# Scores computed transposed, with keys on partitions, in the attention stage of an attention and two-FFN kernel on Trainium2

## The reference

```python
batch, n_heads, seq, head_dim = (4, 8, 576, 64)
q_rot, k_rot = (rotate(q), rotate(k))            # RoPE over halves of 32
scores = np.matmul(q_rot, k_rot.transpose(0, 1, 3, 2)) / np.sqrt(64)
scores = scores - np.max(scores, axis=-1, keepdims=True)
attn = np.exp(scores)
attn = attn / (np.sum(attn, axis=-1, keepdims=True) + 1e-09)
x = np.matmul(attn, v)                           # to [2304 tokens, 512]
x = (x @ w_in1 - np.tanh(x @ w_in1)) @ w_out1    # w_in1 512x2048, w_out1 2048x512
h = x @ w_in2
out = (h * (1.0 / (1.0 + np.exp(-h)))) @ w_out2
```

## Time and profile before

| | before |
|---|---|
| median of 3 runs | 1187.12 us (1184.62 to 1188.59) |
| profiled execution, first to last instruction | 1186.9 us |
| PE busy | 1118.7 us, 94% |
| PE weight loads busy | 1043.8 us, 88% |
| DVE busy | 610.9 us, 51% |
| ACT busy | 521.9 us, 44% |
| POOL busy | 263.0 us, 22% |
| moved by DMA | 50.86 MB |

### The profile page before, as it was taken

How to read it: one execution, slowest core, us unless ns; L and a number is a source line. 1 busy time by engine, 2 the same in 40 slices (tenths; PEclk the granted TensorE clock), 3 DMA queues, 4 the chain that set the end, 5 groups by cost and what they waited for, 6 DMA issues and landing times.

```text
span 1186.9 us, 18468 instructions
## 1 busy us (share of the span) xinstructions
PE 1118.7 (94%) x6560; PEld 1043.8 (88%) x6560; DVE 610.9 (51%) x969; ACT 521.9 (44%) x1128; POOL 263.0 (22%) x171
## 2 busy tenths in 40 slices
PE   2899999999988899999999999999999999999998
PEld 2778888888868899999999999989998989989897
DVE  5899999999976632322323234762323223232322
ACT  3888989898961232232323232222323222232322
POOL 4556564647145500000000003550000000000000
PEclk9999999999998899999999999989999999999999
DMA  5242423233222300000000000320000000000000
GB/s 174 64 112 68 110 67 106 76 93 89 65 86 84 111 32 1 1 0 0 0 0 0 0 0 29 113 71 1 27 0 27 0 0 27 0 27 0 27 0 27
DMA packets 44493, 50.86 MB, mean 43 GB/s; under 512 B 25376, under 2 KB 25648, under 8 KB 44464
## 3 DMA queue, kind: packets, MB, share of 16 engines
q1 hardware_dynamic: 44464, 50.49, 14.2%
HBM read 36.83 MB, written 4.79 MB: 35 GB/s over the span
## 4 chain that ended last, share of the span: by engine, by line
PE 81%; DVE 6%; DMA 4%; ACT 4%; issue 3%; SPq 1%; POOL 1%; ACTq 0%; DVEq 0%; POOLq 0%
PE ps L557 33%; PE ps L576 17%; PE ps L571 16%; PE ps L443 5%; DMA Vk<-Uk 4%; PE ps L417 3%; PE ps L467 3%; PE ps L468 2%; ACT P L694 2%; PE ps L399 1%; DVE g_l L1029 1%; PE ps L421 1%; DVE negmax L886 1%; DVE pt_l L876 1%; DVE pt_r L881 1%
## 5 line engine op out<-in xcount | busy, mean ns | idle before, releaser
L557 PE MATMUL ps<-xs_h,win_l 128*128 128x384 f32 x768 | 260.7, 339 | 2.7 <-DVE xs_l L946 2.7
L557 PE MATMUL ps<-xs_h,win_h 128*128 128x384 f32 x768 | 259.5, 338 | 0.0
L557 PE MATMUL ps<-xs_l,win_h 128*128 128x384 f32 x768 | 259.2, 337 | 0.0
L822 ACT ACTIVATE g_h<-act 128x384 fp32r<-128x384 f32 x192 | 100.9, 525 | 317.5 <-PE ps L576 133.1
L816 ACT ACTIVATE act<-ps 128x384 f32<-128x384 f32 x192 | 94.4, 492 | 246.0 <-PE ps L557 245.9
L557 PEld LDWEIGHTS ps<-xs_h,win_l 128*128 128x128 f32 x768 | 146.0, 190 | 9.3 <-issue 5.8
L1029 DVE TENSOR_TENSOR g_l<-act,g_h 128x384 fp32r<-128x384 f32 x96 | 85.7, 893 | 130.9 <-ACT g_h L822 130.9
L557 PEld LDWEIGHTS ps<-xs_l,win_h 128*128 128x128 f32 x768 | 145.8, 190 | 3.4
L557 PEld LDWEIGHTS ps<-xs_h,win_h 128*128 128x128 f32 x768 | 145.7, 190 | 0.0
L571 PE MATMUL ps<-g_h,wout_l 128*128 128x384 f32 x384 | 129.9, 338 | 9.1 <-DVE g_l L1029 9.1
L1032 DVE SCALAR_TENSOR_TENSOR g_l<-act,g_h 128x384 fp32r<-128x384 f32 x96 | 60.1, 626 | 139.6 <-ACT g_h L822 139.6
(11 more groups left out here) (79 smaller groups left out, 1926.1 us busy)
## 6 DMA issues: line engine op xcount, KB each, us to landing
Vk<-Uk SPq DMA_DIRECT2D x30, 288.0 KB, 3.7
w_stage<-w_in SPq DMA_DIRECT2D x8, 1024.0 KB, 5.0
w_stage<-w_out SPq DMA_DIRECT2D x8, 1024.0 KB, 5.0
raw_q<-q SPq DMA_DIRECT2D x16, 288.0 KB, 3.8
raw_k<-k SPq DMA_DIRECT2D x16, 288.0 KB, 4.3
out<-ostage SPq DMA_DIRECT2D x5, 768.0 KB, 3.5
vr<-v SPq DMA_DIRECT2D x32, 80.0 KB, 2.8
R<-inverse_sums SPq DMA_DIRECT2D x16, 144.0 KB, 2.7
```

The source lines that it names most:

```text
L557: last = mm(o, w[g][:, kk, c:c + 128], x[:, kk, :], start=(n == 0), stop=(n == 11))
L822: nc.scalar.activation(g_h[f % 2][:, :], act[f % 2][:, :], ACT.Copy, scale=(1.0, 0.5)[L]).then_inc(s_gh, 1)
```

## The change

The whole attention stage is rewritten. The FFN stage, its weights' order and its tiles are unchanged; only the two staging buffers of the weights moved to memory that attention used.

- Scores are computed with keys on partitions and queries along the free axis (`scores`, line 428). P comes out in the form in which `pv` wants it, so P is not transposed any more. A pair is 9 units of 128 keys.
- q and k are read from the input already transposed, together with a copy whose halves are exchanged, so RoPE (`rope_scale`, `rope_add` on POOL) needs no transposes and no exchange of halves; the input `qk` has 4 rows of 576 per partition and pair.
- Since the maximum is over keys, which are now on partitions, a product of the high parts alone is formed in the old orientation one pair ahead (`row_scores`, line 403, 2 matmuls a unit), DVE takes its maxima (line 668), PE transposes the 9 columns of maxima (line 409), ACT copies them to a row (line 575) and two small DMAs per head write them as a 65th contraction row of q (`max_rows`, lines 231 and 233), against a row of ones in k. The score matmul then yields score minus maximum.
- P is split without a copy: `exps` (lines 590 and 591) takes the exponential twice, once into the fp32r high part, once back into PSUM in fp32; `low` (DVE, line 676) subtracts.
- V is stored as 128 columns: 64 of values and 64 of ones, so that the same matmul gives the sums (`weigh`, lines 453 to 455: high times high, high times low, low times high, 6 matmuls a unit).
- The operands of the matmuls are stacked in SBUF by DMAs: `stack_high` (4 DMAs a pair, two of them a row of zeros) and `stack_cross` (4 DMAs a pair).
- The sums are gathered by DMA, inverted on DVE, stored and read back spread as before.

Core of the diff (new lines; the functions they replace are listed above):

```diff
+            def stack_high(n):
+                if n >= 3:
+                    sp.wait_ge(s_st, 9 * (n - 2))
+                sp.wait_ge(s_hq, n + 1)
...
+                for h in range(2):
+                    sp.dma_start(t[64:65, h, Q, data(h)].bitcast(F32).rearrange("p (a c) -> p a c", a=9),
+                                 zrow[:, :, :].bitcast(F32).to_broadcast([1, 9, 64])).then_inc(s_tb, 16)
+                    sp.dma_start(t[0:64, h, :, data(h)].bitcast(F32),
+                                 hl[64 * h:64 * h + 64, QH:KH + 1:2, :].bitcast(F32)).then_inc(s_tb, 16)
...
+            for n in range(PAIRS):
+                if n + 1 < PAIRS:
+                    stack_cross(n + 1)
+                if n + 3 < PAIRS:
+                    load(n + 3)
+                max_rows(n, 1)
+                if n >= 1:
+                    gather_sums(n - 1, 1)
+                    join_heads(n - 1)
+                if n + 2 < PAIRS:
+                    stack_high(n + 2)
+                if n >= 1:
+                    store_inverse(n - 1)
+                    spread_inverse(n - 1)
+                if n + 1 < PAIRS:
+                    load_v(n + 1)
+                gather_sums(n, 0)
+                if n + 1 < PAIRS:
+                    max_rows(n + 1, 0)
+                if n >= PAIRS - 2:
+                    load_w(n - (PAIRS - 2))
...
+            for n in range(PAIRS):          # POOL
+                if n + 2 < PAIRS:
+                    qk_low(n + 2)
+                else:
+                    weight_low(n - (PAIRS - 2))
+                if n + 1 < PAIRS:
+                    v_low(n + 1)
+                if n + 3 < PAIRS:
+                    rope_scale(n + 3)
+                if n >= 1:
+                    normalise(n - 1)
+                if n + 3 < PAIRS:
+                    rope_add(n + 3)
...
+            for n in range(PAIRS):          # PE
+                for u in range(9):
+                    if n + 1 < PAIRS:
+                        row_scores(n + 1, u)
...
+                    scores(n, u, extra)
+                    weigh_slot(9 * n + u - 2)
...
+            def qk_high(n):
+                if n == 0:
+                    sc.wait_ge(s_r0, 2)
+                else:
+                    sc.wait_ge(s_rope, n)
+                    sc.wait_ge(s_tb, 64 * n)
+                    sc.wait_ge(s_ta, 64 * n)
...
+            for n in range(PAIRS):          # ACT
+                for u in range(9):
...
+                    exps(n, u, extra)
+                    if u == 3 and n + 2 < PAIRS:
+                        qk_high(n + 2)
+                    if u == 5 and n + 1 < PAIRS:
+                        v_high(n + 1)
...
+                for u in range(9):          # DVE
+                    if n + 1 < PAIRS:
+                        row_max(n + 1, u)
+                    low(9 * n + u - 1)
+                    if u == 1:
+                        move_out(n - 1, 1)
+                    if u == 4:
+                        invert(n - 1)
+                    if u == 6:
+                        move_out(n, 0)
```

More of the change, by code:

```diff
@@ L58, in attention_and_two_ffn @@
         shared = cursor[0]
+        stage = [place(f"w_stage{i}", [128, 4, 512]) for i in range(2)]
         xs_h = place("xs_h", [128, 4, TN], F32R)
@@ L82, in attention_and_two_ffn @@
[L82 to L90, removed]
@@ L296, in _ @@
-            run_pairs(sp, body)
-            load_w(2)
-            load_w(3)
-            spread_inverse(lambda per: per * PAIRS)
-            for w in range(4, 4 * NG):
+            stack_high(0)
+            stack_cross(0)
+            load(2)
+            max_rows(0, 0)
+            stack_high(1)
+            for n in range(PAIRS):
[19 more added lines that the diff above has]
+                    load_w(n - (PAIRS - 2))
@@ new lines, in weigh @@
+            def weigh(n, u, part=None):
+                g = 9 * n + u
+                h, i = S_UNITS[u]
+                if part is not None:
+                    h = part
+                slot = 2 * i + h
+                first = (i == 0) if h == 0 else (i == REST)
+                final = (i == REST) if h == 0 else (i == 3)
+                pe.wait_ge(s_lo, g + 1)
+                if first:
+                    pe.wait_ge(s_vl, n + 1)
+                    if h == 0:
+                        if due(n):
+                            pe.wait_ge(s_ev[1], n)
+                    else:
+                        pe.wait_ge(s_ev[0], n + 1)
+                a, b = vh[n % 2][:, slot, :], vl[n % 2][:, slot, :]
+                for half in range(2):
+                    c = slice(HALF * half, HALF * half + HALF)
+                    o = ps[:, OB + half, 0:HALF]
+                    mm(o, a, ph[g % RING][:, c], start=first, stop=False)
+                    mm(o, b, ph[g % RING][:, c], start=False, stop=False)
+                    last = mm(o, a, pl[g % RING][:, c], start=False, stop=final)
+                if final:
+                    last.then_inc(s_o[h], 1)
+                if part != 0 and not final:
+                    last.then_inc(s_pv, 1)
@@ new lines, in _ @@
+            for j in range(9):
+                row_max(0, j)
+            for n in range(PAIRS):
+                for u in range(9):
[8 more added lines that the diff above has]
+                        move_out(n, 0)
+                    if n >= PAIRS - 2 and u == 8:
+                        weight_high(n - (PAIRS - 2))
```

985 lines of the change are left out of this document (368 added, 617 removed).

## The result

The change as made takes 1278.32 us (median of 4 runs, 1269.2 to 1285.05) against 1186.3 beside it: ratio 1.0767, 95% interval 1.0717 to 1.0817. It is **slower by 92 us**. The prediction was 1240 with a range of 1188 to 1280, so the direction and the kind of cause were right, the size was 38 us short, and the range holds the result by 1.7 us only. The profiled execution spans 1273.7 us; its own time is 1275.79. Of the six runs of e12_act_rows_alone further down, three (1295 to 1303 us) count as slow ones and are left out of its row; its ratio is of the other three.

A forecast was written before the change was run, and what follows sets the result against it. SP's order delays v, so ACT's loop (9.85 + 13.0 us) plus 1.4 for the clock gives 24.3 us a pair. Attention sums to 415 us against 359.21, +56, FFN -3: 1187 + 53 = 1240 us, range 1188 to 1280.

The forecast's parts named there:

- PE, ACT and DVE fit: Steady attention pair: PE's work 16.3 us, ACT 13.6, DVE 14; about 17.5 us a pair if nothing else spoke.
- SP's order binds: SP's list in each pair: v's load stands behind stacking, inverse and spreads, so ACT stands still about 6 us.
- POOL's loop: From v's arrival through POOL's low part of v, normalise and RoPE's addition to the next q and k copy: 22.5 us a pair.
- Lands just as ACT gets to unit 4, so I cost it at nothing: Second maxima row, max_rows(n, 1), behind 2.4 MB in the queue: arrives in time for unit 4, cost nothing.
- Only the maxima's row is late: Rival: max_rows(n, 1) lands about 9.6 us into a pair, wanted at 7.9; pair 19.2 us, 1180 us in all; 4%.
- Four stacking copies, 2.0 us: SP's issues after the q and k copy: two small at 0.31, two large at 0.60, with gaps 2.0 us.
- The store of the inverse: SP's list behind stacking: the store and its return, 1.24 us on an empty queue plus 0.6, 1.85 in all.
- from a to v's high part: a is when qk_high(n+2) ends on ACT, after unit 3; v's high part was put at a + 9.85 us.
- 1.4 us for the half clock behind v: PE idles over 6 us in ACT's loop and its clock falls towards 1.2 GHz: 1.4 us added a pair.
- The rest of the sum: Up to the first FFN matmul: first scores 34, pair 0 20, pair 14 22, pair 15 18, then 5; total 415 us.
- FFN -3: FFN stage: loses a little less waiting for its weights, -3 us, between -8 and +5.
- the rival with more contention: Rival: each DMA in the chain lands 1 us later, PE stays slow longer; pair 28 us, 1288 us in all; 10%.

The follow-up runs named there:

- e12_act_rows_alone: Against the change as made: only the maxima's rows are issued by ACT on its own queue instead of by SP; 1274.47 us, ratio 1.0703.
- e11_act_rows: Maxima's rows issued by ACT, on a kernel with SP's order mended, DVE's inversion earlier and both ends of attention changed (1183.16 us); 1163.5 us.
- e1_v_early: Against the change as made: SP issues the next pair's v load right after the second maxima rows; 1269.62 us, period 24.70.
- e2_max_early: Against the change as made: SP issues second maxima rows, sums' gather and joining of heads ahead of the 1.18 MB q and k load; 1301.56 us.
- e4_warm: Against the change as made: 45 added matmuls, results thrown away, ahead of unit 4 of every pair but the first; 1285.0 us, ratio 1.0817.
- e7_no_zero: Against the kernel with SP's order mended (1191.87 us): copies of zeros removed, row scores contract 64 rows instead of 65; 1214.35 us.

## Why the prediction was right, and where it was short

- **PE, ACT and DVE fit (right).** With SP's order mended, pairs take 17.2 us at best (187.56, 204.76 and 222.00 are consecutive copies of q and k in e11_act_rows), where the prediction had 17.5 for the engines alone and 16.3 for PE.
- **SP's order binds (right).** The place was right: e12_act_rows_alone shows ACT waiting 8.0 us for v in each of 13 pairs, the prediction said 6. POOL's loop, 22.5 us a pair in the prediction, never was the last: in the change as made RoPE's addition ends at 216.20, and the copy of q and k that needs it starts at 218.12 behind ACT's own work. Line 561 never waits for POOL.
- **"Lands just as ACT gets to unit 4, so I cost it at nothing" (wrong).** PE stood for the rows 5.2 us a time. In the change as made this hid the v chain nearly wholly, so the sign that I had named, waits of some 6 us on line 570, isn't there (25.5 us in 14). That the period came out near the forecast all the same is luck: it could leave out the rows because their chain is a second one that is 0.34 us shorter. The rival "Only the maxima's row is late" had priced that chain at 19.2 us a pair where e1_v_early shows 24.70, taking 8.1 us for the queue; issues of 1.30 and 1.13 us behind it weren't in that.
- **Four stacking copies, 2.0 us:** 3.0 (193.67 to 196.66). The row of zeros costs 0.79 to issue, not 0.31 as in the earlier trace rows.
- **The store of the inverse:** costed as ready when SP comes. It was 1.77 us late, since the sums come back behind the load. The return was 1.44, not 1.85. v's landing was 3.5, near the 3.8 of the earlier trace rows; the 2.75 worked out in the prediction from the Trainium skill ("DMA: Bandwidth & Descriptors", Anatomy of one DMA), for its software path, was too short here. In all 11.7 us from a to v's high part, not 9.85, in this pair and in the mean of the 13 from 46.05 us on.
- **1.4 us for the half clock behind v (not in the chain here).** The drop came as predicted, and a low clock behind v does cost 1.4 us or more a pair, as e12_act_rows_alone and e2_max_early show. But as the rows were late, PE went through it ahead of v, and e4_warm found nothing to gain. From v's high part to the next a it is 12.6 to 14.05 us, 13.35 in the mean, where the prediction had 13.0 + 1.4. So 11.70 and 13.35 make up the mean pair, **25.04 against 24.3**: 1.85 more up to v and 1.05 less behind it, two misses that offset each other in part.
- **The rest of the sum.** From the first exponential of one pair to that of the next, pairs 1 to 13 take (391.13 - 61.58) / 13 = 25.35, 1.05 more than predicted and 13.7 in all. The first score matmul is at 37.10, not 34, as each of the nine rounds took 1.70 us and not 1.3: 3.1. The two matmuls of a round take 0.85 us up to the end and start 0.24 us apart as at the low clock, though the profile's clock column reads 1.00 there; this pace lasts to 47.08 us, inside pair 0. The prediction had the low clock in the steady pairs and left it out here. Pair 0 took 22.9, not 20: 2.9. Pair 15 and what follows took 31.2 (412.77 to 444.0), not 23: 8.2, two waits of 3.46 and 4.35 us for weights and a split of x of 3.72 us beside POOL, where the one before the first FFN took 1.76 in the kernel before. From first matmul to first exponential, 1.6. Pair 14, 21.6, was right. These make 29 us, 444 against 415.
- **FFN -3:** it was +2. 1240 + 29 + 5 is the measured 1274.

Of the 38 us missing, the pairs made 14, both ends 15 and the FFN 5; the rest is that the median is 4.6 us above the span of the profiled execution. The 45% of the prediction lay on 1228 to 1262; the result is outside of that, nearer to the rival with more contention (1288, 10%), whose premise, DMAs in the chain landing later, holds for the sums and the store, while its pair of 28 us doesn't.

## What to carry to other kernels

A small transfer that someone waits for must not be issued behind a large one that nobody waits for yet; look for it on the queue's list, since engines' busy shares don't show it. When two chains of nearly the same length close over a loop, a single edit doesn't show what it is worth: one took off 9 us, one added 23, both together took off 55. A low clock costs only where PE is in the chain. And price the first and last rounds of a pipeline from their own dependencies, not as steady rounds.

## What the runs showed of the hardware that was not expected

- With 64 contraction rows among matmuls of 65 and 128 PE takes some 0.37 us longer for a unit of 12, 1.98 against 1.61; with 65 rows, one of them zeros, the gap isn't there (e7_no_zero, 22 us; that the rows are the cause is argued, not shown).
- A DVE instruction of 9 columns, SBUF to SBUF, takes 2.63 us beside a POOL instruction of 2.65, while the maxima and the low parts, which read PSUM, keep their 0.75 us beside POOL. The split of x, all in SBUF, took 3.72 us beside POOL and 1.76 otherwise, and POOL's `normalise` beside it 2.92 instead of 1.43.
- A DMA of 4.5 KB comes back in 4.07 us behind a load of 1152 KB in the same queue, in 1.44 where that load is older.
- An issue on SP takes longer right behind large ones, for copies of one shape: `tb<-rows` is 0.69 and 0.55 us in one place of a pair (207.32, 208.06) and 1.30 and 1.13 in the other (189.00, 190.34), behind four copies of 288 KB and a load of 1152 KB.
